# Attention scores in three single-pass products of high and low parts, from the third unit on

## The reference, cut to what matters

```python
def _attn_ref(q, k, v, alpha):          # (4, 8, 768, 48) each
    state = zeros((B, H, D, D))
    for t in range(S):
        state = alpha[:, :, t, :, None] * state + einsum('bhd,bhe->bhde', k[:, :, t], v[:, :, t])
        y[:, :, t] = einsum('bhd,bhde->bhe', q[:, :, t], state)
    return y

def _moe_ref(x, g_ln, w_ch1, w_ch2):    # x (4, 768, 384), w_ch1 (384, 1536)
    xn = (x - mean) / sqrt(var + 1e-06) * g_ln
    return x + maximum(xn @ w_ch1, 0.0) @ w_ch2

def _moe2_ref(x, w_ch1, w_ch2):
    u = x + real(fft(fft(x, axis=1), axis=2))
    un = (u - mean) / sqrt(var + 1e-06)
    return u + maximum(un @ w_ch1, 0.0) @ w_ch2
```

## Time and profile before

| | |
|---|---|
| median of 3 runs | 801.92 us (801.89 to 803.3) |
| the profiled execution's own time | 801.9 us |
| its span in the profile | 800.4 us |
| PE busy | 789.9 us (99%) |
| PEld busy | 780.3 us (97%) |
| DVE busy | 459.1 us (57%) |
| ACT busy | 239.2 us (30%) |
| POOL busy | 74.2 us (9%) |
| granted clock of PE, mean | 0.999 of full speed |

### The profile page before, as it was taken

The page is one execution under the profiler, slowest core; times in us unless marked ns, Lnnn a source line. Parts: engine busy times, 40 slices in busy tenths (PEclk is TensorE's granted clock), DMA queues, the critical chain, the costliest instruction groups (busy, mean ns, idle before and its releaser), DMA issues.

```text
span 800.4 us, 13050 instructions
## 1 busy us (share of the span) xinstructions
PE 789.9 (99%) x4934; PEld 780.3 (97%) x4934; DVE 459.1 (57%) x1013; ACT 239.2 (30%) x450; POOL 74.2 (9%) x117
## 2 busy tenths in 40 slices
PE   7999999999999999999999999999999999999998
PEld 6899999999999999999999999999999999999998
DVE  7994756647747657376476785436633464342322
ACT  4452332232413322323334423212221222211211
POOL 2224000000000000000000500210012000300000
PEclk9999999999999999999999999999999999999999
DMA  9634232042032141423304511120001200000000
GB/s 199 156 92 122 55 80 40 30 90 43 17 88 59 40 102 47 96 64 99 129 16 133 193 64 51 50 99 31 1 30 44 85 0 0 29 0 31 1 30 30
DMA packets 60299, 51.37 MB, mean 64 GB/s; under 512 B 26460, under 2 KB 59996, under 8 KB 60252
## 3 DMA queue, kind: packets, MB, share of 16 engines
q1 hardware_dynamic: 60252, 50.74, 23.2%
HBM read 41.29 MB, written 13.37 MB: 68 GB/s over the span
## 4 chain that ended last, share of the span: by engine, by line
PE 94%; DVE 4%; issue 0%; DMA 0%; POOL 0%; ACT 0%; DVEq 0%
PE h L44 13%; PE h L46 12%; PE h L45 12%; PE acc L46 12%; PE acc L44 12%; PE acc L45 12%; PE side_bank L1274 5%; PE side_bank L1310 5%; PE side_bank L1306 2%; PE side_bank L1318 2%; PE side_bank L45 2%; PE side_bank L46 2%; PE side_bank L1287 1%; PE side_bank L44 1%; PE side_bank L1258 1%; DVE F_inv L921 1%
## 5 line engine op out<-in xcount | busy, mean ns | idle before, releaser
L121 DVE SCALAR_TENSOR_TENSOR hT_low<-h,hT_high 128x384 fp32r<-128x384 f32 x192 | 106.5, 555 | 191.0 <-ACT hT_high L116 190.7
L44 PE MATMUL h<-xnT_high,w_high 128*128 128x384 f32 x576 | 205.0, 356 | 0.5 <-DVE xnT_low L992 0.3
L116 ACT ACTIVATE hT_high<-h 128x384 fp32r<-128x384 f32 x192 | 94.4, 492 | 348.6 <-PE h L46 348.6
L44 PE MATMUL acc<-w_high,hT_high 128*128 128x384 f32 x576 | 193.7, 336 | 0.0
L46 PE MATMUL h<-xnT_high,w_low 128*128 128x384 f32 x576 | 193.7, 336 | 0.0
L45 PE MATMUL h<-xnT_low,w_high 128*128 128x384 f32 x576 | 193.5, 336 | 0.0
L46 PE MATMUL acc<-w_high,hT_low 128*128 128x384 f32 x576 | 192.8, 335 | 0.0
L45 PE MATMUL acc<-w_low,hT_high 128*128 128x384 f32 x576 | 192.4, 334 | 0.0
L44 PEld LDWEIGHTS h<-xnT_high,w_high 128*128 128x128 f32 x576 | 108.5, 188 | 1.9 <-issue 0.5
L45 PEld LDWEIGHTS h<-xnT_low,w_high 128*128 128x128 f32 x576 | 108.6, 188 | 1.1
L45 PEld LDWEIGHTS acc<-w_low,hT_high 128*128 128x128 f32 x576 | 108.2, 188 | 0.0
(11 more groups left out here) (118 smaller groups left out, 838.0 us busy)
## 6 DMA issues: line engine op xcount, KB each, us to landing
stage<-w_dram SPq DMA_DIRECT2D x24, 384.0 KB, 3.3
v_pad<-v_dram SPq DMA_DIRECT2D x16, 288.0 KB, 5.4
x_scratch<-x_unit SPq DMA_DIRECT2D x8, 576.0 KB, 3.0
a_in<-alpha_dram SPq DMA_DIRECT2D x7, 576.0 KB, 4.9
q_in<-q_dram SPq DMA_DIRECT2D x7, 576.0 KB, 6.9
k_in<-k_dram SPq DMA_DIRECT2D x7, 576.0 KB, 8.5
xb<-x_scratch SPq DMA_DIRECT2D x4, 576.0 KB, 4.0
xb<-x_turned SPq DMA_DIRECT2D x4, 576.0 KB, 6.8
```

The costliest lines, as they stand in the source:

```text
L44: pe.matmul(out, wh, xh, start=start, stop=False)
L116: act.activation(self.hT[0][:, j % H_SLOTS, :], self.hps[j % H_BANKS][:, 0:UN], ACT.Relu).then_inc(self.h_high, 1)
L121: dve.scalar_tensor_tensor(out=self.hT[1][:, j % H_SLOTS, :], in0=self.hps[j % H_BANKS][:, 0:UN], scalar=0.0, in1=self.hT[0][:, j % H_SLOT ...
```

## The change

For units 0 and 1 the scores stay as they are (`in_fp32`). From unit 2 on ACT writes the spread q as `q_diag_high` (fp32r), and a new step `round_k` writes `k_part_high` (fp32r) from `k_div`. A new step `split_qk` on DVE makes `q_diag_low` with two instructions (q_mul times the head's row mask, minus `q_diag_high`) and `k_part_low` with one. `scores` then makes each product with `split_matmul`, three fp32r products of 256 columns in place of one in full fp32. The first score half waits for `qk_split` in place of `k_ready` and `q_diag_ready`.

The four new tiles, and `q_whole` of units 0 and 1 (which shares their room), hold one chunk each in place of three. So ACT's `spread_q` waits until the scores of the chunk before are summed, and is moved: for chunk 1 and 2 from slots 2 and 4 to slots 3 and 6, behind `copy_y` (in unit 1 chunk 1 stays in slot 2). `round_k` stands behind it, for the next unit's chunk 0 in slot 11. `split_qk` stands in slots 0, 3 and 6 on DVE.

```diff
-            q_diag = sb1("q_diag", [R, PAIRS, UT, 2, P])
+            with ExitStack() as shared:
+                q_whole = sb("q_whole", [R, 2, PAIRS, 2, P], where=shared)
+            q_diag = [sb1(f"q_diag_{p}", [R, PAIRS, 2, P], F32R) for p in ("high", "low")]
+            k_part = [sb1(f"k_part_{p}", [R, PAIRS, P], F32R) for p in ("high", "low")]
...
+        def in_fp32(n):
+            return isinstance(n, int) and n < 2
+        def splits_before(n, c):
+            return UT * (n - 2) + c
...
@@ ACT
+                if not (first(n) and c == 0):
+                    act.wait_ge(sc_summed, 2 * (UT * n + c))
                 for two in range(2):
-                    op = act.activation(q_diag[:, :, c, two, :], q_mul[:, :, c, :], ACT.Copy,
+                    to = q_whole[:, 0, :, two, :] if in_fp32(n) else q_diag[0][:, :, two, :]
+                    op = act.activation(to, q_mul[:, :, c, :], ACT.Copy,
                                         scale=head_rows[:, two:two + 1])
                 op.then_inc(q_diag_ready, 1)
+            def round_k(n, c):
+                act.wait_ge(k_ready, UT * n + c + 1)
+                act.wait_ge(sc_summed, 2 * (UT * n + c))
+                act.activation(k_part[0][:, :, :], k_div[:, :, c, :], ACT.Copy).then_inc(k_rounded, 1)
...
-                if slot in (2, 4):
-                    spread_q(n, slot // 2)
+                if in_fp32(n) and slot == 2:
+                    spread_q(n, 1)
                 if slot in (3, 6, 9):
                     copy_y(n, slot // 3 - 1, par)
+                if slot in (3, 6) and not (in_fp32(n) and slot == 3):
+                    spread_q(n, slot // 3)
+                    if not in_fp32(n):
+                        round_k(n, slot // 3)
...
+                if slot == 11 and more:
+                    round_k(n + 1, 0)
@@ DVE
+            def split_qk(n, c):
+                q = splits_before(n, c)
+                dve.wait_ge(q_diag_ready, UT * n + c + 1)
+                for two in range(2):
+                    dve.scalar_tensor_tensor(out=q_diag[1][:, :, two, :], in0=q_mul[:, :, c, :],
+                                             scalar=head_rows[:, two:two + 1], in1=q_diag[0][:, :, two, :],
+                                             op0=ALU.mult, op1=ALU.subtract)
+                dve.wait_ge(k_rounded, q + 1)
+                dve.tensor_tensor(k_part[1][:, :, :], k_div[:, :, c, :], k_part[0][:, :, :],
+                                  ALU.subtract).then_inc(qk_split, 1)
...
+                if slot == 0 and not in_fp32(n):
+                    split_qk(n, 0)
                 if slot in (0, 3):
                     prepare_q(n, 1 + slot // 3)
+                if slot in (3, 6) and not in_fp32(n):
+                    split_qk(n, slot // 3)
@@ PE, scores
-                if half == 0:
+                if half == 0 and in_fp32(n):
                     pe.wait_ge(k_ready, UT * n + c + 1)
                     pe.wait_ge(q_diag_ready, UT * n + c + 1)
+                elif half == 0:
+                    pe.wait_ge(qk_split, splits_before(n, c) + 1)
...
+                    if in_fp32(n):
+                        op = pe.matmul(to, k_div[:, 2 * half + h, c, :], qs[0], start=True, stop=True)
+                    else:
+                        op = split_matmul(pe, to, [k[:, 2 * half + h, :] for k in k_part], qs, True, True)
```

More of the change, by code:

```diff
@@ L270, in spare @@
             def spare(i):
-                rows = q_diag[:, i // UT, i % UT, :, :].rearrange("p two t -> p (two t)")
+                rows = q_whole[:, 0, i, :, :].rearrange("p two t -> p (two t)")
                 return rows[:, 0:PAIRS * D].rearrange("p (h e) -> p h e", h=PAIRS)
             step_v, step_state, step_product, step_head = (spare(i) for i in range(4))
-            step_in = q_diag[:, 2, 0, 0, 0:3 * PAIRS].rearrange("p (i h) -> p i h", i=3)
-            step_out = q_diag[0:1, 3, 0:2, :, :].rearrange("p c two t -> p (c two t)")[:, 0:2 * PAIRS * D].rearrange(
+            step_in = q_whole[:, 1, 2, 0, 0:3 * PAIRS].rearrange("p (i h) -> p i h", i=3)
+            step_out = q_whole[0:1, 1, 0:2, :, :].rearrange("p c two t -> p (c two t)")[:, 0:2 * PAIRS * D].rearrange(
                 "p (two h e) -> p two h e", two=2, h=PAIRS)
@@ L329, in pipeline @@
         q_diag_ready = sem("q_diag_ready")
+        k_rounded = sem("k_rounded")
+        qk_split = sem("qk_split")
         kT_summed = sem("kT_summed")
@@ L1273, in scores @@
                 for h in range(2):
-                    op = pe.matmul(score_bank(n, half)[:, h * 2 * P:(h + 1) * 2 * P], k_div[:, 2 * half + h, c, :],
-                                   q_diag[:, 2 * half + h, c, :, :].rearrange("p two t -> p (two t)"),
-                                   start=True, stop=True)
+                    to = score_bank(n, half)[:, h * 2 * P:(h + 1) * 2 * P]
+                    qs = [q[:, 2 * half + h, :, :].rearrange("p two t -> p (two t)")
+                          for q in ([q_whole[:, 0, :, :, :]] if in_fp32(n) else q_diag)]
+                    if in_fp32(n):
+                        op = pe.matmul(to, k_div[:, 2 * half + h, c, :], qs[0], start=True, stop=True)
+                    else:
+                        op = split_matmul(pe, to, [k[:, 2 * half + h, :] for k in k_part], qs, True, True)
                 op.then_inc(sc_summed, 1)
```

## The result

| | before | changed |
|---|---|---|
| median | 801.9 us | 813.7 us (813.69 to 814.12) |
| span of the profiled execution | 800.4 us | 812.2 us |
| granted clock, mean | 0.999 | 1.0 |

The changed kernel is slower: 1.0144 of the time before, with an interval of 1.0126 to 1.0161. Forecast were 813.3 us. Medians are compared unless a run at full clock is named: single executions at a granted clock of 0.995 to 0.998, of the kernel before too, are 0.5 to 1.6 us longer than those at full clock.

The account below looks back on a forecast made before the run. PE was taken to bound the kernel, busy 789.9 of 800.4 us. From 801.9 us, passes gave -6.1 and waits for the split +17.5, making 813.3 us; range 806 to 820, its own terms' bounds 808.9 to 821.

Parts of the forecast that it names:

- What bounds it: Whole kernel: PE, busy 789.9 of 800.4 us; DVE and ACT don't matter until PE waits for them.
- The passes: Score halves on PE: six passes of 0.120 us replace 0.89 us, gaining 0.17 in each of 36, -6.1 us.
- Rival D: Score passes on PE: the three passes gain nothing, 0.148 us each, 819.4 us; chance 0.04.
- The split: `split_qk` on DVE: three instructions of 0.67, 0.67 and 0.69 us, 2.03 us until the last is done.
- Rivals A and B: `split_qk` on DVE at double rate: two scalar instructions, 801.6 us, chance 0.04; or all three, 798.9 us, chance 0.04.
- The waits: PE waits for the split in slots 1, 4 and 7, 2.76 or 3.08 us a unit, +17.5 us together.
- Slot 1: Chunk 0's scores: PE's products start at 201.54 against 200.09, a wait of 1.45 us.
- Slot 7: Chunk 2's scores: PE waits 0.60 us in first halves of a sequence, 0.92 in second halves.
- Slot 4: Chunk 1's scores: a chain of 3.91 us from `copy_y` against PE's 3.20, a wait of 0.71 us.
- What was put at nothing: Other moved steps on DVE, ACT and SP, such as `prepare_q`, low parts, masks and loads, cost PE no time.
- the cover of slot 3: DVE's `prepare_q` in slot 3 ends 0.6 us before chunk 1's spread q comes, so it adds no wait.
- rival C: Slots 3 and 4: the chain slips further, about 1 us more in 6 units, 819.3 us; chance 0.10.

Follow-up runs that it names:

- the version without waits: Changed kernel with chunk 0's split at the end of slot 11, spread and rounding before `copy_y`, DVE's split before `prepare_q`: 797.0 us, 0.9937 of before.
- the one-pass kernel: Changed kernel with only the first, high by high, of each score product's three passes made: 796.5 us, 0.993 of before.

## Why the prediction was right

**What bounds it.** Right. Only what PE did or waited for moved the time: 34 us more on DVE cost nothing in the version without waits, and 11 more there cost nothing again. The busier engines were forecast at 38 and 11 us for DVE and ACT, and the page has 34.4 and 7.8. The new groups do add up to 25.3 + 12.2 = 37.5 and to 11.2, but the next instruction starts up to 0.1 us before the shown end of the one before, and the page counts that time once.

**The passes.** The step chose 0.120 us for a pass of 256 columns; the starts in the trace are 0.12 apart and the one-pass kernel gives 0.120. What was a little off is the price of the old half, 0.89 forecast and 0.87 measured, so that a half gained 0.156 where 0.17 stood: 5.6 us in place of 6.1. The rule of the Trainium skill's page "TensorE: Matmul & The Clock Gate" (Back-to-back issue gap), 109 ns, is 11 low for this stream of passes. Rival D (0.148 a pass) falls.

**The split.** 2.03 us forecast, 2.00 measured. The scalar operand costs what its like had cost in the network's low part: (204.77 - 203.45) / 2 = 0.66 each, against 0.67. Rivals A and B needed 0.34. The nearest row, of the same form with two tensors, was the right one and the clamp of one tensor the wrong one.

**The waits.** All of them: 17.5 forecast, 17.3 to 17.4 by the experiments at full clock. Slot 1: 1.45 forecast, 1.46 measured. Slot 7: 0.60 and 0.92 forecast for first and second halves, 0.65 and 0.98 measured on average. Slot 4: 0.71 forecast, 0.69 on average, and that is in part luck. The step took PE's 3.20 us after `copy_y` from one first half for all six units; in the second halves and in the last first half PE asked at 3.29 to 3.31, which takes 0.4 us from the sum. Against that, waking PE cost more than the 0.12 of the step: in slots 4 and 7 of the loop PE started 0.13 behind the split's end (219.86 to 219.99), in slot 1 and in the units that are written out 0.05 (389.03 to 389.08), and the first pass costs 0.11 more in place of 0.07. So two errors of opposite sign lie in this term. Read wait by wait the rows give 17.8, about 0.5 more than the experiments, and each unit ran 0.06 to 0.09 shorter than its three waits less its gain add up to; which row gives that back I haven't found.

**What was put at nothing.** Right: PE's waits for `hT_low` and `probs` are those of before (0.2 and 0.7 us in all), the cover of slot 3 held (DVE waited 0.59 there), rival C didn't come. One wait wasn't priced ahead: in unit 1 of the attention, beside the first unit of the network, ACT waits 2.9 us for the scores of the chunk before. The step had said only that PE has room there, and PE indeed didn't notice.

**The sum.** 813.3 against 813.7; in spans +11.8 against +11.4. The forecast as a whole stood on two terms, and the experiments show each by itself: +17.3 to +17.4 for the waits, -5.5 to -5.6 for the passes. The 0.4 us by which it missed are mostly the smaller gain of the passes.

**Slips in the working that didn't touch the forecast.** The upper end adds up to 821.7, not 821, and a cover of 0.6 us lost in six units would be 3.6 and not 2, so it should have been 823. The split at which waits and gain cancel is 1.39 by the step's own waits, not 1.36. The waits were to show as 17 us in the profile, which has 13.1: its idle time leaves out the 0.26 at each.

## What to carry to other kernels

When one engine fills its span, a cheaper operand form is worth what it saves only if its operands are still ready when that engine asks for them. So add up the chain from the last thing that the preparing engine must wait for, and compare it with the time at which the full engine asks, in every kind of unit and not in one. Here the arithmetic gained 5.6 us, and the places in which the preparation stood cost 17.4; two moves, one slot earlier on DVE and ahead of a copy on ACT, took the cost away and left the gain. The same added instruction cost its full length (0.66 us) 18 times on the chain, and nothing beside it, so look for a place ahead of a wait that its engine has anyway.

## What the runs showed of the hardware

**PE's clock fell behind waits of some 2 us.** With one more instruction in the split, PE waits 1.86 us in slot 1. In the profiled execution the granted clock fell to half, the 1.2 GHz level, at or shortly after the end of such waits. The wait:

```profile
94.15 0.38 PE L44 MATMUL side_bank<-q_diag_high,k_part_high 96*128 96x256 f32 x1 [1.86 <-DVE k_part_low L991]
```

The stretches behind it (stretch, length, busy us and count of PE, PEld, DVE, ACT, POOL, granted clock, DMA share, GB/s):

```profile
92.00:94.00 2.00, 0.28 (x4) 0.10 (x2) 2.00 (x4) 0.86 (x2) 0.00 (x0) 1.00 0.56 204
94.00:96.00 2.00, 1.85 (x12) 1.85 (x13) 1.87 (x6) 0.00 (x0) 0.00 (x0) 0.97 0.00 0
96.00:98.00 2.00, 2.00 (x8) 2.00 (x7) 1.41 (x4) 0.49 (x1) 0.00 (x0) 0.50 0.04 8
98.00:100.00 2.00, 2.00 (x12) 1.99 (x11) 0.41 (x1) 0.00 (x0) 0.00 (x0) 0.68 0.00 0
100.00:102.00 2.00, 2.00 (x18) 2.00 (x17) 1.43 (x3) 0.00 (x0) 0.00 (x0) 1.00 0.00 0
```

Here PE stands, works again at full clock for about 2 us, and then has the half clock for about 3 (8 matmuls in a stretch in place of 12 or more), though it is busy throughout. In the next unit, where PE is back at 153.86, the clock is down as soon as it is back:

```profile
154.00:156.00 2.00, 2.00 (x9) 2.00 (x10) 1.87 (x6) 0.00 (x0) 0.00 (x0) 0.50 0.00 0
```

A fall of the clock came in all six units of that execution, (835.2 - 825.6) / 6 = 1.6 us each, and not at all in the run of 825.6 us, whose clock was full. The waits of slots 4 and 7 in it, and the waits of the changed kernel (1.20 shown at most), had none of it.

With two more instructions, a longer wait kept the clock in one place and a shorter one lost it in another, in slot 4:

```profile
95.87 0.39 PE L44 MATMUL side_bank<-q_diag_high,k_part_high 96*128 96x256 f32 x1 [2.64 <-DVE k_part_low L996]
...
111.78 0.43 PE L44 MATMUL side_bank<-q_diag_high,k_part_high 96*128 96x256 f32 x1 [1.98 <-DVE k_part_low L996]
```

```profile
96.00:98.00 2.00, 2.00 (x14) 2.00 (x15) 1.87 (x6) 0.00 (x0) 0.00 (x0) 1.00 0.00 0
110.00:112.00 2.00, 0.22 (x1) 0.23 (x2) 2.00 (x4) 0.33 (x1) 0.00 (x0) 0.99 0.00 0
112.00:114.00 2.00, 2.00 (x9) 2.00 (x9) 0.80 (x3) 0.00 (x0) 0.00 (x0) 0.50 0.00 0
114.00:116.00 2.00, 2.00 (x9) 2.00 (x9) 1.90 (x9) 0.10 (x1) 0.00 (x0) 0.65 0.00 0
```

Over the profiled execution (860.2 us) the clock fell in ten places: at four of the six waits of slot 1 (2.64 us), five of the six of slot 4 (1.78 to 1.98) and one of the six of slot 7 (1.78 to 2.19). What decides which of these waits costs the clock stays open: its length alone doesn't. None of it touches the changed kernel's result, whose clock was full, but it makes waits of about 2 us dearer than their length.
